# Both batches' scores first, then two parts of the network, at each level

## The chip, the cores and the metric

The kernel runs on 1 core of one Trainium2 chip. The metric is the device time of an execution in microseconds (us), the median of the runs. The core's engines work side by side, each through its own list of instructions in order: TensorE (PE; its weight loads are listed as PEld), VectorE (DVE), ScalarE (ACT), GpSimd (POOL) and SyncE (SP), which here only starts transfers. They wait for one another on semaphores.

## What is computed

A linear attention with a decaying state (4 batches, 8 heads, 768 steps, 48 channels a head), then two gated networks on the 3072 tokens of 384 channels. Everything is float32.

```python
for t in range(S):                     # the attention
    cur = einsum('bhd,bhe->bhde', u * kt, vt)
    y[:, :, t] = einsum('bhd,bhde->bhe', rt, state + cur)
    state = wt[..., None] * state + einsum('bhd,bhe->bhde', kt, vt)

xn = x / sqrt(mean(x * x) + 1e-6) * rms_g        # first network, width 1536
x  = (silu(xn @ w_gate) * (xn @ w_val)) @ w_out
h  = maximum(maximum(x @ w1, x @ w2), x @ w3)    # second network, width 768
out = h @ w_out2
```

## The kernel before

**Tiles and levels.** The 768 steps are cut into 6 tiles of 128. In a tile the attention of two batches at a time, a duo, is worked out in 7 levels by doubling: at level l the 128 steps are blocks of 2h = 2^(l+1), and the right half of each block sees its left half. `rB[j]` holds batch j's r (j is 0 or 1 in the duo; two rows of partitions hold the even and the odd heads), `kT[b]` its k, `wT[b]` the decays of the blocks. Per level and batch:

- TensorE's `scores` (L503) multiplies kT with the right halves of rB into the bank `ps_sc[:, j]`, eight matmuls for four pairs of heads; level 0 has none. It waits for both rescales of the level before and for the copy of the level before out of the same bank.
- VectorE's `rescale_r_even` (L913) and GpSimd's `rescale` (L1168 for k, L1175 for the odd heads' r) multiply by the block's decay. They wait for the level's scores and for the block decays of the level before.
- VectorE's `take_scores` (L938, at the last level L946) copies the scores that belong to the level into `A`, masked.
- VectorE's `double_blocks` (L925) makes the decays of the doubled blocks; it waits for all three rescales.

After the last level come the transposes of k (`k_token_major`, L540), the output (`attended`, L522 and L527), the update of the state (L549), and VectorE's terms for a token and its neighbour (`own_term`, `neighbour_term`; the latter behind levels 4 and 5). GpSimd multiplies r and k (`r_times_k`, L1146) behind level 5.

**The slots.** The first network for the tile before is spread over the attention. Its 36 parts come in threes for each of 12 columns f of the hidden layer: gate (f), value (f), output (f - 1), nine matmuls each (L484 to L486, each product split into three of high and low halves). A duo has 18 slots, two at each level (2l and 2l + 1) and four behind them, and each slot takes the next part. `part` exists on four engines: ScalarE makes the sigmoid of the gate (L703) and the high half of the hidden values (L707), VectorE the products with gate (L888, which frees the gate's bank) and value (L891), GpSimd the low half (L1139). All engines run the slots in the same order, and what stands in an engine's list ahead of a step holds it up. Tile 0 has no network yet in its first duo; there ScalarE and VectorE split weight pieces in some slots (`weights_early`; L876, L878). In tile 0's second duo each slot has two parts, on 256 tokens, and a weight piece with each odd part; tile 1's parts too have 256 tokens, those of later tiles 512. Slot 0 of tile 0's second duo also makes the transposed and split x (L741, L1040). The tiles 2 to 4 are one loop. After the last tile come the remaining pass of the first network and the second network.

**What sets the order.** The order is written out by hand in each engine's `duo_steps`. On TensorE and GpSimd a level is: batch 0's scores (or rescale), slot 2l, batch 1's, slot 2l + 1. On VectorE: rescale and copy of batch 0, slot 2l, rescale and copy of batch 1, doubling of batch 0, slot 2l + 1, doubling of batch 1.

Of the kernel before, what the change touches and what calls it, by code (L numbers as in the profile page):

```python
# [45 lines left out]
def rwkv_moe_kernel(nc, rc, kc, wc, r, k, v, u, g_w1, v_w1, o_w1, rms_g, w1, w2, w3, o_w2, out):  # L46
# [17 lines left out]
    with ExitStack() as ctx:  # L64
# [178 lines left out]
        def k_nth(a, duo, level, j):  # L243

            return step(duo, level, j) + 1 - (2 * duo if last_tile(a) else 0)
# [233 lines left out]
        def _(pe):  # L479
# [8 lines left out]
            def scores(a, duo, level, j):  # L488
                if level == 0:
                    return  # L490
                h = 1 << level
                after(pe, r_even_scaled, a, STEPS, r_nth(a, duo, level - 1, j))
                after(pe, r_odd_scaled, a, STEPS, r_nth(a, duo, level - 1, j))
                after(pe, k_scaled, a, STEPS, k_nth(a, duo, level - 1, j))
                if level == 1 and duo and last_tile(a):
                    after(pe, scores_used, a, SCORES, score(duo - 1, LEVELS - 1, j) + 1)
                elif level == 1:
                    after(pe, u_taken, a, B, 2 * duo + j - 1)
                else:
                    after(pe, scores_used, a, SCORES, score(duo, level, j) - 1)  # L500
                for q in range(PAIRS):
                    rights = rB[j][:, :, q, :].rearrange("p o (n two h) -> p o n two h", two=2, h=h)[:, :, :, 1, :]
                    last = mm(ps_sc[:, j, q * T:(q + 1) * T], kT[2 * duo + j][:, q, :], rights, start=True, stop=True)  # L503
                last.then_inc(scores_done, 1)
# [101 lines left out]
            def duo_steps(a, duo, slot):  # L606
                for level in range(LEVELS):
                    for j in range(2):
                        scores(a, duo, level, j)
                        slot(2 * level + j)  # L610
                k_token_major(a, duo, 0)
                k_token_major(a, duo, 1)
                attended(a, duo, 0)
                slot(TAIL_AT)
                state_update(a, duo, 0)
                attended(a, duo, 1)
                slot(TAIL_AT + 1)
                state_update(a, duo, 1)
                slot(TAIL_AT + 2)
                slot(TAIL_AT + 3)  # L620
# [57 lines left out]
        def _(act):  # L678
# [73 lines left out]
            def duo_steps(a, duo, slot):  # L752
                for level in range(LEVELS):
                    for j in range(2):
                        if level == LEVELS - 1:
                            copy_r_left(a, duo, j)
                        slot(2 * level + j)
                k_back(a, duo, 0)
                k_back(a, duo, 1)
                slot(TAIL_AT)  # L760
                squares(a, duo, 0)
                slot(TAIL_AT + 1)
                squares(a, duo, 1)
                slot(TAIL_AT + 2)
                slot(TAIL_AT + 3)
# [100 lines left out]
        def _(dve):  # L866
# [175 lines left out]

            def duo_steps(a, duo, slot):
                for level in range(LEVELS):
                    rescale_r_even(a, duo, level, 0)
                    take_scores(a, duo, level, 0)
                    slot(2 * level)
                    rescale_r_even(a, duo, level, 1)
                    take_scores(a, duo, level, 1)
                    double_blocks(a, duo, level, 0)  # L1050
                    slot(2 * level + 1)
                    double_blocks(a, duo, level, 1)
                    if level in NEIGHBOURS_AT:
                        neighbour_term(a, duo, NEIGHBOURS_AT.index(level))
                own_term(a, duo, 0)
                slot(TAIL_AT)
                add_y(a, duo, 0)
                decay_state(a, duo, 0)
                add_to_state(a, duo, 0)
                normalise(a, duo, 0)  # L1060
                own_term(a, duo, 1)
                slot(TAIL_AT + 1)
                add_y(a, duo, 1)
                decay_state(a, duo, 1)
                slot(TAIL_AT + 2)
                normalise(a, duo, 1)
                add_to_state(a, duo, 1)
                slot(TAIL_AT + 3)
# [62 lines left out]
        def _(pool):  # L1131
# [52 lines left out]
            def duo_steps(a, duo, slot):  # L1184
                for level in range(LEVELS):
                    for j in range(2):
                        rescale(a, duo, level, j)
                        slot(2 * level + j)
                    if level == LEVELS - 2:
                        r_times_k(a, duo, 0)  # L1190
                times_u(a, duo, 0)
                r_times_k(a, duo, 1)
                times_u(a, duo, 1)
                slot(TAIL_AT)
                inverse_rms(a, duo, 0)
                slot(TAIL_AT + 1)
                inverse_rms(a, duo, 1)
                slot(TAIL_AT + 2)
                slot(TAIL_AT + 3)
# [78 lines left out]
```

## Time and profile before

| | |
|---|---|
| median of 3 runs | 1040.18 us (1038.83 to 1042.09) |
| the profiled execution | 1042.37 us, span 1040.6 us, mean granted clock 0.985 |
| TensorE busy | 997.7 us (96%), 5680 matmuls |
| TensorE weight loads | 882.3 us (85%) |
| VectorE | 623.3 us (60%) |
| ScalarE | 246.2 us (24%) |
| GpSimd | 489.2 us (47%) |

Times in the rows are counted from the span's start. A busy share is an average over stages with different limits, so the stretches matter: the attention fills the first 650 us, in which VectorE and GpSimd have most of their work. A row of the timeline gives start, duration, engine, line, operation, output and inputs, shapes and count; in brackets the idle time before it and what ended it, where there was some.

### The profile page before, as it was taken

Reading aid. Unit: us, or ns where it says so; the run is one execution under the profiler, and the core shown is the slowest. Engines: PE = TensorE matmul, PEld = TensorE weight load, DVE = VectorE, ACT = ScalarE, POOL = GpSimd, SP = SyncE. Lnnn points to the kernel's source line nnn. Section 1 sums busy time; section 2 is a strip of 40 time slices with the busy share of each in tenths; the row PEclk is TensorE's granted clock in tenths of the full one; section 3 lists DMA queues with packets and bytes.
Section 4 is the critical chain, followed back from the end, with each engine's and each line's share of the span. In section 5 each row is a group of like instructions: output and inputs, shape, how many; then the busy total and the mean of one; then the engine's idle time right before and its main releaser. Section 6 shows DMA issues by size and latency. Waiting matters only on the chain.

```text
span 1040.6 us, 16737 instructions
## 1 busy us (share of the span) xinstructions
PE 997.7 (96%) x5680; PEld 882.3 (85%) x5680; DVE 623.3 (60%) x1047; ACT 246.2 (24%) x488; POOL 489.2 (47%) x540
## 2 busy tenths in 40 slices
PE   4778988899999999999999999999999999999998
PEld 4778988888888888888888888888888888888988
DVE  7878798988776877778776867444332212121221
ACT  2132312222123121222122212333322212121211
POOL 7656586857574757566674757212010201011111
PEclk9689999999999999999999999999999999999999
DMA  6533312212112120303021220201301010101000
GB/s 200 161 89 96 97 46 77 74 50 96 58 60 63 55 97 3 108 12 133 18 88 34 91 63 5 92 31 61 122 0 61 1 61 8 53 15 45 23 8 31
DMA packets 36221, 64.65 MB, mean 62 GB/s; under 512 B 4928, under 2 KB 22720, under 8 KB 36160
## 3 DMA queue, kind: packets, MB, share of 16 engines
q1 hardware_dynamic: 30288, 52.12, 15.2%
q10 hardware_dynamic: 5872, 11.80, 3.5%
q8 instruction: 28, 0.46, 0.2%
q14 instruction: 33, 0.27, 0.1%
HBM read 54.46 MB, written 9.44 MB: 61 GB/s over the span
## 4 chain that ended last, share of the span: by engine, by line
PE 84%; DVE 5%; POOL 5%; issue 3%; ACT 1%; DMA 0%; SPq 0%; ACTq 0%; POOLq 0%; DVEq 0%
PE ps_sc L503 10%; PE ps_acc L484 8%; PE ps_acc L486 8%; PE ps_acc L485 8%; PE ps_gate L484 6%; PE ps_gate L486 6%; PE ps_val L484 6%; PE ps_gate L485 6%; PE ps_val L486 5%; PE ps_val L485 5%; PE ps_desk L527 3%; PE ps_sc L486 2%; PE ps_sc L484 2%; PE ps_sc L485 2%; POOL kT L1168 2%
## 5 line engine op out<-in xcount | busy, mean ns | idle before, releaser
L503 PEld LDWEIGHTS ps_sc<-rB,kT 128*128 128x128 f32 x1152 | 155.8, 202 | 36.8 <-DVE rB L913 18.0
L503 PE MATMUL ps_sc<-rB,kT 128*128 128x128 f32 x1152 | 162.2, 288 | 25.8 <-DVE A L938 10.6
L1168 POOL TENSOR_TENSOR kT<-kT,wT 128x256 f32<-128x256 f32 x164 | 140.0, 853 | 83.9 <-PE ps_sc L503 56.4
L1236 POOL TENSOR_TENSOR h_lo<-h2f,h_hi 128x512 fp32r<-128x512 f32 x36 | 46.3, 1285 | 247.5 <-ACT h_hi L857 247.5
L1139 POOL TENSOR_TENSOR h_lo<-act_h,h_hi 128x512 fp32r<-128x512 f32 (+1 forms) x83 | 97.7, 1178 | 108.8 <-ACT h_hi L707 104.2
L1175 POOL TENSOR_TENSOR rB<-rB,wT 64x256 f32<-64x256 f32 x144 | 121.1, 841 | 11.3
L913 DVE TENSOR_TENSOR rB<-rB,wT 64x256 f32<-64x256 f32 x144 | 96.1, 672 | 30.4 <-PE ps_sc L503 23.7
L484 PE MATMUL ps_gate<-x_hi,wg_hi 128*128 128x512 f32 (+1 forms) x252 | 97.0, 385 | 8.9 <-DVE act_h L888 6.9
L707 ACT ACTIVATE h_hi<-act_h 128x512 fp32r<-128x512 f32 (+1 forms) x84 | 47.9, 571 | 230.4 <-DVE act_h L891 230.2
L938 DVE COPY_PREDICATED A<-mask,ps_sc 128x512 f32<-128x512 uint8 x120 | 98.9, 824 | 0.0
L484 PE MATMUL ps_acc<-h_hi,wo_hi 128*128 128x512 f32 (+1 forms) x252 | 95.7, 380 | 0.5 <-POOL h_lo L1139 0.3
L484 PE MATMUL ps_val<-x_hi,wv_hi 128*128 128x512 f32 (+1 forms) x252 | 96.2, 382 | 0.0
L703 ACT ACTIVATE act_h<-ps_gate 128x512 f32<-128x512 f32 (+1 forms) x84 | 45.1, 536 | 212.8 <-PE ps_gate L486 212.6
L486 PE MATMUL ps_gate<-x_hi,wg_lo 128*128 128x512 f32 (+1 forms) x252 | 91.8, 364 | 0.0
L486 PE MATMUL ps_val<-x_hi,wv_lo 128*128 128x512 f32 (+1 forms) x252 | 91.7, 364 | 0.0
L485 PE MATMUL ps_gate<-x_lo,wg_hi 128*128 128x512 f32 (+1 forms) x252 | 91.2, 362 | 0.0
L485 PE MATMUL ps_val<-x_lo,wv_hi 128*128 128x512 f32 (+1 forms) x252 | 91.1, 362 | 0.0
L925 DVE TENSOR_TENSOR wT<-wT 128x128 f32<-128x128 f32 (+6 forms) x160 | 77.1, 490 | 23.4 <-POOL rB L1175 21.5
L486 PE MATMUL ps_acc<-h_hi,wo_lo 128*128 128x512 f32 (+1 forms) x252 | 90.9, 361 | 0.0
L485 PE MATMUL ps_acc<-h_lo,wo_hi 128*128 128x512 f32 (+1 forms) x252 | 90.5, 359 | 0.0
L1115 DVE TENSOR_TENSOR h2f<-h2f,ps_val 128x512 f32<-128x512 f32 x18 | 12.4, 688 | 106.2 <-PE ps_val L486 106.2
L891 DVE TENSOR_TENSOR act_h<-act_h,ps_val 128x512 f32<-128x512 f32 (+1 forms) x84 | 51.4, 612 | 35.4 <-PE ps_val L486 34.1
(136 smaller groups left out, 2028.7 us busy)
## 6 DMA issues: line engine op xcount, KB each, us to landing
kT<-in_k_channels SPq DMA_DIRECT2D x24, 256.0 KB, 3.4
wT<-in_w_channels SPq DMA_DIRECT2D x24, 256.0 KB, 4.0
rB<-in_r_channels SPq DMA_DIRECT2D x48, 128.0 KB, 2.6
kL<-in_k_tokens SPq DMA_DIRECT2D x24, 192.0 KB, 2.4
rL<-in_r_tokens SPq DMA_DIRECT2D x24, 192.0 KB, 2.5
vL<-in_v_tokens SPq DMA_DIRECT2D x24, 192.0 KB, 2.4
x_scratch<-x1s SPq DMA_DIRECT2D x6, 768.0 KB, 4.4
xn<-x_scratch SPq DMA_DIRECT2D x6, 768.0 KB, 4.3
```

Of the source, the lines that this page charges most:

```text
L484: mm(dst, lhs[0], rhs[0], start=start, stop=False)
L485: mm(dst, lhs[0], rhs[1], start=False, stop=False)
L486: return mm(dst, lhs[1], rhs[0], start=False, stop=stop)
L503: last = mm(ps_sc[:, j, q * T:(q + 1) * T], kT[2 * duo + j][:, q, :], rights, start=True, stop=True)
L707: nc.scalar.activation(h_hi[:, f % 2, toks], act_h[:, f % 2, toks], ACT.Copy).then_inc(h_hi_done, 1)
L891: tt(hidden, hidden, ps_val[:, toks], ALU.mult).then_inc(val_used, 1)
L913: tt(new, old, block_decay(2 * duo + j, 1 << level, 0, HEAD_ROWS[0]), ALU.mult).then_inc(r_even_scaled, 1)
L925: tt(left, left, half(w[:, :, :], h, 1)[:, :, 0:1], ALU.mult).then_inc(tot_done, 1)
L938: nc.vector.copy_predicated(dst, every_head.broadcast_to([P, H, n, h]), src.rearrange("p (g n h) -> p g n h", g=H, h=h)).then_inc(scores_u ...
L1139: tt(h_lo[:, f % 2, toks], act_h[:, f % 2, toks], h_hi[:, f % 2, toks].bitcast(F32), ALU.subtract).then_inc(h_lo_done, 1)
L1168: tt(half(kT[b][:, :, :], h, 0), half(kT[b][:, :, :], h, 0), block_decay(b, h, 1), ALU.mult).then_inc(k_scaled, 1)
L1175: tt(new, old, block_decay(b, h, 0, HEAD_ROWS[1]), ALU.mult).then_inc(r_odd_scaled, 1)
```

## The change

In each engine's `duo_steps` the two batches' steps of a level come first and the level's two slots behind them. On VectorE the doublings of both batches also come ahead of both slots. On ScalarE the two copies of r (last level alone) come ahead of the last level's two slots. Instructions, waits and buffers are the same; only their order in the lists changes.

```diff
--- before
+++ after
@@ TensorE, duo_steps @@
                 for level in range(LEVELS):
                     for j in range(2):
                         scores(a, duo, level, j)
+                    for j in range(2):
                         slot(2 * level + j)
@@ ScalarE, duo_steps @@
                     for j in range(2):
                         if level == LEVELS - 1:
                             copy_r_left(a, duo, j)
+                    for j in range(2):
                         slot(2 * level + j)
@@ VectorE, duo_steps @@
                 for level in range(LEVELS):
-                    rescale_r_even(a, duo, level, 0)
-                    take_scores(a, duo, level, 0)
-                    slot(2 * level)
-                    rescale_r_even(a, duo, level, 1)
-                    take_scores(a, duo, level, 1)
-                    double_blocks(a, duo, level, 0)
-                    slot(2 * level + 1)
-                    double_blocks(a, duo, level, 1)
+                    for j in range(2):
+                        rescale_r_even(a, duo, level, j)
+                        take_scores(a, duo, level, j)
+                    for j in range(2):
+                        double_blocks(a, duo, level, j)
+                    for j in range(2):
+                        slot(2 * level + j)
@@ GpSimd, duo_steps @@
                     for j in range(2):
                         rescale(a, duo, level, j)
+                    for j in range(2):
                         slot(2 * level + j)
```

## Rows read from the trace of the kernel before

**Rows 1.** Windows: start:end, length, then busy us (instructions) of PE, PEld, DVE, ACT, POOL; clock.

```profile
83.00:86.50 3.50, 3.50 (x20) 3.50 (x19) 2.66 (x4) 2.02 (x3) 2.63 (x3) 0.54 0.43 123
...
174.00:222.70 48.70, 43.62 (x351) 41.87 (x352) 42.72 (x81) 11.92 (x30) 34.23 (x42) 1.00 0.21 66
336.20:449.70 113.50, 113.50 (x673) 99.42 (x673) 87.56 (x155) 26.48 (x54) 72.09 (x80) 1.00 0.19 63
```

**Rows 2.** Waits of TensorE: waiter, releaser, us in total, times, longest.

```profile
PE ps_sc L503 <- DVE A L938: 10.6, 7, 3.1
...
PE ps_gate L484 <- DVE act_h L888: 6.9, 5, 1.9
```

**Rows 3.** Timeline of TensorE in tile 3: start us, us, engine, line, op, tiles, count.

```profile
336.26 1.98 PE L503 MATMUL ps_sc<-rB,kT 128*128 128x128 f32 x16
337.99 0.48 PE L484 MATMUL ps_gate<-x_hi,wg_hi 128*128 128x512 f32 x1
...
340.17 1.05 PE L503 MATMUL ps_sc<-rB,kT 128*128 128x128 f32 x8
340.97 0.48 PE L484 MATMUL ps_val<-x_hi,wv_hi 128*128 128x512 f32 x1
...
369.81 1.03 PE L540 MATMUL ps_sc<-ident,kT 128*128 128x128 f32 x8
...
386.12 0.39 PE L484 MATMUL ps_gate<-x_hi,wg_hi 128*128 128x512 f32 x1
...
388.16 0.39 PE L484 MATMUL ps_val<-x_hi,wv_hi 128*128 128x512 f32 x1
```

**Rows 4.** Timeline of all engines in tile 3, first duo, levels 1 and 2.

```profile
340.93 1.31 DVE L938 COPY_PREDICATED A<-mask,ps_sc 128x512 f32<-128x512 uint8 x1
...
345.33 0.69 DVE L891 TENSOR_TENSOR act_h<-act_h,ps_val 128x512 f32<-128x512 f32 x1
...
346.06 0.63 ACT L707 ACTIVATE h_hi<-act_h 128x512 fp32r<-128x512 f32 x1 [5.10 <-DVE act_h L891]
...
346.76 1.29 POOL L1139 TENSOR_TENSOR h_lo<-act_h,h_hi 128x512 fp32r<-128x512 f32 x1 [0.36 <-ACT h_hi L707]
```

**Rows 5.** Timeline of VectorE in tile 1, second duo, levels 2 and 3.

```profile
182.58 0.42 DVE L891 TENSOR_TENSOR act_h<-act_h,ps_val 128x256 f32<-128x256 f32 x1
182.91 0.41 DVE L913 TENSOR_TENSOR rB<-rB,wT 64x256 f32<-64x256 f32 x1
...
184.82 0.86 DVE L925 TENSOR_TENSOR wT<-wT 128x64 f32<-128x64 f32 x1 [0.71 <-POOL rB L1175]
```

**Rows 6.** Timeline of GpSimd in tile 1, second duo, levels 0 to 5.

```profile
174.80 0.92 POOL L1175 TENSOR_TENSOR rB<-rB,wT 64x256 f32<-64x256 f32 x1
...
184.81 0.74 POOL L1139 TENSOR_TENSOR h_lo<-act_h,h_hi 128x256 fp32r<-128x256 f32 x1
...
187.11 0.85 POOL L1168 TENSOR_TENSOR kT<-kT,wT 128x256 f32<-128x256 f32 x1
...
188.78 0.65 POOL L1168 TENSOR_TENSOR kT<-kT,wT 128x256 f32<-128x256 f32 x1
...
198.94 1.49 POOL L1146 TENSOR_TENSOR prod<-rL,kL 128x384 f32<-128x384 f32 x1
```

**Rows 7.** Timeline of TensorE in tile 1, second duo: scores and transposes.

```profile
183.30 1.06 PE L503 MATMUL ps_sc<-rB,kT 128*128 128x128 f32 x8
...
191.25 1.06 PE L503 MATMUL ps_sc<-rB,kT 128*128 128x128 f32 x8
...
202.26 0.66 PE L540 MATMUL ps_sc<-ident,kT 128*128 128x128 f32 x4 [1.05 <-DVE A L946]
```

**Rows 8.** Timeline of GpSimd in tile 0, first duo: an odd rescale.

```profile
26.22 1.57 POOL L1175 TENSOR_TENSOR rB<-rB,wT 64x256 f32<-64x256 f32 x1
```

**Rows 9.** Timeline of all engines in tile 0, second duo, level 0.

```profile
57.71 0.55 PE L484 MATMUL ps_gate<-x_hi,wg_hi 128*128 128x256 f32 x1 [0.98 <-ACT x_hi L741]
...
63.20 0.95 DVE L913 TENSOR_TENSOR rB<-rB,wT 64x256 f32<-64x256 f32 x1
```

## The prediction

> **What bounds the kernel now.** I read the windows first. In tile 3, which stands for the tiles 2 to 5, TensorE is busy for 113.5 of 113.5 us and VectorE for 87.6 [rows 1]: TensorE is the bound, and the reader should see that the other engines have some 20% of slack, no more. In the second half of tile 1 (its network parts work on 256 tokens instead of 512) the picture turns: VectorE is busy for 42.7 of 48.7 us, close to TensorE's 43.6 [rows 1]. There and in tile 0 the bound changes from level to level. The list of TensorE's waits says on whom: 10.6 us in 7 places for the copies of the scores (L938), 6.9 us in 5 places for the gate product of VectorE (L888) that frees the gate's bank [rows 2]. So the thing to look at is not how much work there is, which the change leaves alone, but what stands in front of what in the queues of VectorE and GpSimd, and how much slack each has.
>
> **The order on TensorE itself, tiles 2 to 5.** From the scores at 340.17 to the transposes at 369.81 there are ten pairs of one batch's scores and one part: 29.64 / 10 = 2.964 us a pair, 5.93 us a level [rows 3]. One batch's scores alone take 0.80 us (340.17 to 340.97). In the new order a level is both scores, a part behind them, and a part behind a part. All three are in the trace, because in the first duo one slot is empty and level 0 has no scores: both scores take 337.99 - 336.26 = 1.73 us (not 2 x 0.80: the first part overlaps the tail of the scores before it only once), a part behind scores 340.17 - 337.99 = 2.18, a part behind a part 388.16 - 386.12 = 2.04 [rows 3]. Sum 5.95 against 5.93: +0.02 to +0.03 a level. Changed levels of such kind: 5 in a first duo (level 1 is already paired there), 6 in a second, 11 a tile, 44 in four tiles: **+1.2 us**. If the part behind a part keeps its gain and the paired scores cost nothing extra, it is -0.12 x 44 = -5.3; that is the lower end.
>
> **The waits that appear in tiles 2 to 5.** Scores (2,1), level 2 of batch 1, now start 0.80 us behind those of (2,0) instead of 2.96. They need the copy of scores (1,1) out of the same bank. In tile 3 that copy runs from 340.93 for 1.31 us [rows 4], at the end of two rescales and two copies that VectorE does in one go. In the new order the doubling of level 0 is out of their way and GpSimd's low part no longer meets them, so I take the copy to end at about 341.5, where (2,1) could start at 340.97: +0.5 us in a first duo. In a second duo the same place gives +0.3. Four tiles: 4 x 0.8 = **+3.2**, between 0 (the rescale of batch 1 may run alone, 0.41 us, instead of beside GpSimd, 0.95 [rows 5, 9], and that closes the gap) and 8 (the whole step of 1.3 in first and 0.7 in second duos). Elsewhere in the level the slack holds, narrowly. GpSimd needs 188.78 - 187.11 = 1.67 us for a batch's two rescales [rows 6], so both are done 0.9 + 3.34 = 4.2 us after the level begins, and scores (l+1,1) want them at 5.95 + 0.80 = 6.75. The low part of the hidden values, 1.29 us with 512 tokens [rows 4], stands between the levels when VectorE has made the value product, which is now queued behind the doubling of batch 1, which waits for GpSimd's last rescale: 4.2 + 0.3 + two products of 0.69 + ScalarE's 0.63 [rows 4] = 6.5, then 1.3, and GpSimd starts the next level's rescales at 7.8 instead of 6.8. Then their end is 7.8 + 3.34 = 11.1 and the scores (l+2,1) want them at 12.7. So one such level costs nothing, and it comes every third.
>
> **Tile 1.** Here a part is half as long, and the same chain has no slack. From scores (3,0) at 183.30 to (5,0) at 191.25 two levels take 7.95 us, 3.98 each, set by TensorE [rows 7]. I walk the second duo with the durations of the rows. Scores (1,1) wait for GpSimd's rescale of batch 1, which ends at 174.80 + 0.92 = 175.72 [rows 6]: they can't start earlier than today, and the part that stood ahead of them now stands behind, up to +1.1 us. VectorE's products of gate and value, 0.42 us each [rows 5], move behind the doubling. At (2,0) the copy of (1,0) is late by 0.7 and at (2,1) that of (1,1) by 0.3; scores (3,0) come at 184.6 instead of 183.3. In level 2 the doubling of batch 1 waits for GpSimd as it does now (0.71 us of idle time in front of it at 184.82 [rows 5]); but gate and value product, which now fill the place between the two copies (182.58 [rows 5]), come only after it, at 186.1 to 186.9. ScalarE's copy (0.42) and GpSimd's low part (0.74, 184.81 now [rows 6]) end at 188.2, and only then GpSimd takes level 3: scores (4,0) at 189.8 instead of 187.3, +2.5 us. Levels 3 and 4 run at TensorE's rate or 0.5 us above it. In level 5 the same order of waits returns, and behind it stands GpSimd's product of r and k (1.49 us [rows 6]): the low part at 202.0, the product to 204.1, level 6's rescales from 204.1; the transposes begin at 202.26 today [rows 7] and get the second k at 206.6, which puts what follows them 3.3 us later; and the output of the second batch waits 0.4 us more for VectorE: **+3.7 us** for this duo (1 to 5.5). The first duo walked in the same way gives less, since its level 1 is paired already: **+1.7** (0 to 3).
>
> **Tile 0.** In the first duo TensorE has no parts; the change only moves the split of a weight piece (L878) from between the two doublings to behind them. Now it meets GpSimd's rescale of batch 1, which takes 1.57 us [rows 8] instead of 0.92 [rows 6], in the chain that sets the level. Behind the doubling it meets the next level's first rescale, which has more room: about 0.35 us a level for three levels, **-1.0** (-2 to 0). In the second duo each slot has two parts and two weight pieces. The split of x stands in slot 0; today VectorE makes it ahead of batch 1's rescale (63.20 [rows 9]), after the change behind both rescales and both doublings, and the second doubling waits for GpSimd until 57.9. The first gate part then starts at 59.65 instead of 57.71 [rows 9]: +1.9. After that VectorE sets the pace, with the same work; walking it level by level I get its arrival at level 3 within 0.3 us of today's, at level 5 1.3 later, and the transposes at 113.2 instead of 110.9: **+2.3** (-3 to +6). TensorE waits for the gate product in blocks of 3 to 4 us in place of at most 1.9 [rows 2].
>
> **The sum.** -1.0 + 2.3 + 1.7 + 3.7 + 3.2 + 1.2 = +11.1 us. The profiled execution took 1042.4 us (span 1040.6), which is 2.2 above the median of 1040.2; from 1042.4 I get 1053.5, on the median 1051.3. No instruction is added, and ScalarE's and SyncE's programs change nowhere else: SyncE's loads wait for outputs and state updates, which stand behind the last level in both orders.
>
> **A rule weighed.** VectorE's even rescale takes 0.41 us alone and 0.95 beside GpSimd's [rows 5, 9], so 0.5 us is lost where the two meet. The Trainium skill (SBUF — State Buffer, Who interferes with whom) says that a VectorE instruction with two SBUF inputs and a GpSimd instruction that reads SBUF exclude each other for a whole instruction, while one with an SBUF and a PSUM input doesn't contend. By that rule the new order is worse than my walk: it takes the two PSUM products out of the time in which GpSimd rescales and leaves only contending ones there. The trace agrees in direction; in size the loss of 0.5 is less than a whole rescale of GpSimd.
>
> **The rivals.** (a) The order costs nothing measurable: TensorE catches up in tile 1 because the copies come earlier than I walk them, and tile 0's loss is offset by its first duo. -1 + 0 + 1 + 0 + 0 + 1 = +1: 1041. For it speaks VectorE's and GpSimd's slack in tile 3; against it the 0.71 us wait in front of the doubling, which exists today. (b) Faster: parts behind parts at 2.04 us, and the batch 1 scores are no longer held up. Its place is the 44 levels of tiles 2 to 5, its price -5.3, and with -1.0 and -2.0 in tile 0 and nothing lost in tile 1 it gives 1032. It decides if both scores take less than 1.65 us behind one another; the row says 1.73. (c) The clock. In 83.0 to 86.5 TensorE ran at 0.54 of its clock, the 1.2 GHz level for nearly all of it, right behind the wait of 1.9 us [rows 2], and the 3.5 us held what takes about 2 at 2.4 GHz [rows 1]. Waits of 3 to 4 us in tile 0 may bring this two or three times more, at 1.5 us each: 1055. (d) The slack that I found in tiles 2 to 5 is not there: GpSimd falls behind in every third level, as in tile 1, by 0.7 us, and both waits at level 2 last longer. 4 tiles x 2 duos x 2 levels x 0.7 = +11 more: 1062.
>
> **How the numbers follow.** The forecast has 0.50, (a) 0.15, (b) 0.08, (c) 0.15, (d) 0.12. The bounds of the terms reach from 1036 to 1067 if all went one way, which they won't; leaving out (b) and the far half of (d), the range is 1040 to 1061. A measurement of this kernel can tell 0.3%, 3.1 us, from no change. Slower by more: the forecast (its own range is 1044 to 1059), (c) and (d): 0.77. Same: (a), 0.15. Faster: (b), 0.08.
>
> **What would show it.** Right: in tile 3 the pair of scores at 1.73 us and small waits for L938 in front of (2,1), a tile of some 114.6 us; in tile 1 a duo of some 3 us more, with GpSimd's low part right in front of a level's rescales; in tile 0 the first gate part about 2 us later. Wrong: tile 3 unchanged or shorter, or tile 1's waits for L938 gone without others in their place; then VectorE's order mattered less than I think, or the time when GpSimd gets both scores mattered more.

## The result and the profile after

The changed kernel takes 1052.87 us (median; 1052.70 to 1054.77) beside 1041.13 us for the kernel before (1038.83 to 1042.53): a ratio of 1.0119, 95% interval [1.0103, 1.0135]. It is slower by 1.2%. The profiled execution took 1053.0 us, its span is 1051.3 us, 10.7 more than before's 1040.6.

The page of the changed kernel: busy us of each engine, the granted clock of TensorE in 40 slices, and the chain of work that ended last.

```profile
PE 999.4 (95%) x5680; PEld 883.0 (84%) x5680; DVE 635.3 (60%) x1047; ACT 245.9 (23%) x488; POOL 476.1 (45%) x540
...
PEclk9679999999999999999999999999999999999999
...
PE 78%; POOL 9%; issue 6%; DVE 5%; ACT 1%; DMA 0%; POOLq 0%; SPq 0%; DVEq 0%; ACTq 0%
```

The same chain in the kernel before:

```profile
PE 84%; DVE 5%; POOL 5%; issue 3%; ACT 1%; DMA 0%; SPq 0%; ACTq 0%; POOLq 0%; DVEq 0%
```

The same instructions ran, and TensorE is busy nearly as long as before (999.4 and 997.7 us). What has grown is the part of the chain that isn't TensorE: GpSimd's share from 5 to 9%, and the time in which an engine waited for nothing that the profile shows ("issue") from 3 to 6%. To see where, I cut both spans at TensorE's first transposes of x (L564), with which each tile ends. (The lines of VectorE, GpSimd and ScalarE stand one or two lower in the changed kernel: L938 is L940, L925 is L927, L1175 is L1176.)

| stretch, us | before | after | difference | predicted |
|---|---|---|---|---|
| tile 0, first duo | 55.18 | 54.90 | -0.3 | -1.0 |
| tile 0, second duo and tail | 70.64 | 71.28 | +0.6 | +2.3 |
| tile 1 | 89.31 | 94.50 | +5.2 | +5.4 |
| tiles 2 to 4, each | 113.50 | 115.13 | +1.63 | +1.1 |
| tile 5 and the second network | 485.01 | 485.20 | +0.2 | +1.1 |

Windows of the changed kernel (busy us and instructions of PE, PEld, DVE, ACT, POOL; then clock, DMA share, GB/s): the second duo and tail of tile 1, and a tile like tile 3. They answer to the second and third of [rows 1].

```profile
176.20:228.30 52.10, 44.86 (x351) 42.34 (x352) 44.16 (x82) 11.81 (x30) 33.41 (x42) 1.00 0.19 62
343.50:458.50 115.00, 114.11 (x673) 99.76 (x672) 91.39 (x155) 26.45 (x54) 70.53 (x80) 1.00 0.19 62
```

In tile 1 the same 351 matmuls now lie in 52.1 us instead of 48.7, and neither TensorE nor VectorE is full: the time went into waits. TensorE's waits in the changed kernel (us in total, times, longest):

```profile
PE ps_sc L503 <- DVE A L940: 12.2, 11, 4.9
...
PE ps_gate L484 <- DVE act_h L890: 6.6, 4, 3.7
PE ps_sc L503 <- POOL rB L1176: 6.0, 8, 2.1
PE ps_gate L484 <- issue: 3.0, 1, 3.0
...
PE ps_sc L540 <- POOL kT L1169: 1.9, 2, 0.9
...
PE ps_desk L522 <- DVE xn L996: 1.6, 5, 0.5
```

The odd rescale's line in the kernel before:

```profile
PE ps_sc L503 <- POOL rB L1175: 2.5, 3, 1.4
```

Beside [rows 2] the waits for the copies and the gate product have hardly grown in sum. Those for GpSimd's odd rescale went from 2.5 to 6.0 us. New are one of 3.0 us ahead of the first gate part in tile 0 (the profile has no releaser for it), two of 0.95 us of the transposes for GpSimd's k in tile 1, and small ones of the output product (L522) for VectorE at the end of the duos. All of TensorE's waits in this list together went from 39.9 to 48.3 us.

### The profile page after: what moved, and what is told of

It reads as the page before. It is cut to its first block, busy times and chain, and to the rows that moved or that the text cites. A ratio compares the mean times of both kernels' runs of the same rounds, so it can differ in the third digit from the quotient of the medians.

```text
span 1051.3 us, 16735 instructions
## 1 busy us (share of the span) xinstructions
PE 999.4 (95%) x5680; PEld 883.0 (84%) x5680; DVE 635.3 (60%) x1047; ACT 245.9 (23%) x488; POOL 476.1 (45%) x540
## 4 chain that ended last, share of the span: by engine, by line
PE 78%; POOL 9%; issue 6%; DVE 5%; ACT 1%; DMA 0%; POOLq 0%; SPq 0%; DVEq 0%; ACTq 0%
PE ps_sc L503 9%; PE ps_acc L484 7%; PE ps_acc L486 7%; PE ps_acc L485 7%; PE ps_val L484 5%; PE ps_val L486 5%; PE ps_gate L484 5%; PE ps_val L485 5%; PE ps_gate L486 5%; PE ps_gate L485 5%; POOL kT L1169 4%; POOL rB L1176 3%; PE ps_desk L527 3%; PE ps_sc L484 2%; PE ps_sc L486 2%
## 5 line engine op out<-in xcount | busy, mean ns | idle before, releaser
L503 PE MATMUL ps_sc<-rB,kT 128*128 128x128 f32 x1152 | 155.3, 288 | 28.8 <-DVE A L940 12.2
L503 PEld LDWEIGHTS ps_sc<-rB,kT 128*128 128x128 f32 x1152 | 148.6, 201 | 37.9 <-DVE rB L915 18.4
L1169 POOL TENSOR_TENSOR kT<-kT,wT 128x256 f32<-128x256 f32 x164 | 134.8, 822 | 68.2 <-PE ps_sc L503 52.3
L1176 POOL TENSOR_TENSOR rB<-rB,wT 64x256 f32<-64x256 f32 x144 | 113.6, 789 | 11.3
L927 DVE TENSOR_TENSOR wT<-wT 128x128 f32<-128x128 f32 (+6 forms) x160 | 82.2, 528 | 57.4 <-POOL rB L1176 48.8
L915 DVE TENSOR_TENSOR rB<-rB,wT 64x256 f32<-64x256 f32 x144 | 95.3, 668 | 9.9 <-issue 4.5
L940 DVE COPY_PREDICATED A<-mask,ps_sc 128x512 f32<-128x512 uint8 x120 | 98.9, 824 | 0.0
L1116 DVE TENSOR_TENSOR h2f<-h2f,ps_val 128x512 f32<-128x512 f32 x18 | 12.4, 687 | 106.3 <-PE ps_val L486 106.3
L890 DVE TENSOR_TENSOR act_h<-act_h,ps_gate 128x512 f32<-128x512 f32 (+1 forms) x84 | 50.8, 605 | 33.7 <-ACT act_h L704 33.4
```

Source lines behind the costliest of these rows:

```text
L890: tt(hidden, hidden, ps_gate[:, toks], ALU.mult).then_inc(gate_used, 1)
L915: tt(new, old, block_decay(2 * duo + j, 1 << level, 0, HEAD_ROWS[0]), ALU.mult).then_inc(r_even_scaled, 1)
L927: tt(left, left, half(w[:, :, :], h, 1)[:, :, 0:1], ALU.mult).then_inc(tot_done, 1)
L940: nc.vector.copy_predicated(dst, every_head.broadcast_to([P, H, n, h]), src.rearrange("p (g n h) -> p g n h", g=H, h=h)).then_inc(scores_u ...
L1169: tt(half(kT[b][:, :, :], h, 0), half(kT[b][:, :, :], h, 0), block_decay(b, h, 1), ALU.mult).then_inc(k_scaled, 1)
L1176: tt(new, old, block_decay(b, h, 0, HEAD_ROWS[1]), ALU.mult).then_inc(r_odd_scaled, 1)
```

## The experiments

Each kernel changes the order of work and nothing else. They ran in several groups, each with the kernel before beside them (its medians were 1041.13 to 1042.33 us), so the ratios compare better than the times; places inside a kernel are read from its one profiled execution. The theory after the comparison was: the time is lost in VectorE's order, because the doubling of batch 1, which waits for GpSimd's last rescale, now has both products of the network queued behind it. The rivals were TensorE's order itself, VectorE's rescales meeting GpSimd's (contention), and the granted clock of TensorE. The last column is the mean of tiles 2 to 4, between the transposes of x.

| kernel | time, us | ratio to before, 95% | a tile, us |
|---|---|---|---|
| changed kernel | 1052.87 | 1.0119 [1.0103, 1.0135] | 115.13 |
| e1_vector_old | 1041.05 | 0.9993 [0.9983, 1.0003] | 114.35 |
| e3_tensor_old | 1068.93 | 1.0251 [1.0233, 1.0268] | 117.21 |
| e5_doubling_last | 1051.07 | 1.0081 [1.0064, 1.0098] | 114.28 |
| e6_split_first | 1053.13 | 1.0106 [1.0089, 1.0123] | 115.13 |
| e7_tensor_only | 1049.71 | 1.0069 [1.0048, 1.0090] | 115.42 |
| e8_pool_only | 1040.38 | 0.9989 [0.9974, 1.0004] | 113.52 |
| e9_paired_early | 1038.67 | 0.9968 [0.9958, 0.9978] | 113.51 |
| e10_doubling_ahead | 1042.21 | 0.9997 [0.9986, 1.0008] | 114.18 |
| e11_last_level_old | 1049.90 | 1.0080 [1.0063, 1.0097] | 114.40 |
| e12_vector_old_early | 1043.91 | 1.0023 [1.0013, 1.0034] | 115.18 |

**VectorE's order undone.** From the changed kernel:

```diff
-                    for j in range(2):
-                        rescale_r_even(a, duo, level, j)
-                        take_scores(a, duo, level, j)
-                    for j in range(2):
-                        double_blocks(a, duo, level, j)
-                    for j in range(2):
-                        slot(2 * level + j)
+                    rescale_r_even(a, duo, level, 0)
+                    take_scores(a, duo, level, 0)
+                    slot(2 * level)
+                    rescale_r_even(a, duo, level, 1)
+                    take_scores(a, duo, level, 1)
+                    double_blocks(a, duo, level, 0)
+                    slot(2 * level + 1)
+                    double_blocks(a, duo, level, 1)
```

> The change on TensorE, ScalarE and GpSimd, but VectorE's order as it was before (batch 0, slot, batch 1, doubling, slot, doubling). My theory, that VectorE's products queued behind batch 1's doubling (which waits for GpSimd) make the loss of tile 1, expects tile 1's loss of 5.2 us (two duos, +1.9 and +3.3) to shrink to under 2, and the 2.0 us that tile 0's first gate part came later to vanish, since the split of x stands ahead of batch 1's rescale again: 1041 to 1046 us in all. The rival, that the loss comes from TensorE asking for both batches' scores at once, whatever VectorE's order, expects 1050 or more, with the waits of TensorE for L938-like copies in the same places.

Measured: 1041.05 us; the loss is gone. TensorE's order loses nothing on the whole as long as VectorE keeps its own and GpSimd follows. It isn't free everywhere, though: tiles 2 to 4 still take 0.85 us each more than before (114.25 to 114.52), while tile 0 ends 4.7 us earlier (121.13 against 125.82), in part by the clock, as the last run below shows. In the medians gains and losses leave no difference. (The second network, which no kernel here touches, took 1.6 us longer in this one profiled execution than in the others; why, the trace doesn't show.)

**TensorE's order undone**, the other three engines as in the changed kernel:

```diff
                         scores(a, duo, level, j)
-                    for j in range(2):
                         slot(2 * level + j)
```

> The change on VectorE, GpSimd and ScalarE, but TensorE in its old order (batch 0's scores, part, batch 1's scores, part). If VectorE's order makes the loss, it is here in full or more, because batch 1's scores now also come a part later (2.2 us with 512 tokens, 1.1 with 256) and the doubling and both products wait for them: 1053 to 1075 us, with TensorE waiting for the gate product in most levels of tile 1. If asking for both scores at once makes the loss, this kernel loses nothing: 1039 to 1044 us.

Measured: 1068.93 us, worse than both. VectorE waits in the middle of its level for the scores of batch 1, which TensorE makes one part later, and now has no product to do meanwhile: both stand behind that wait. A tile takes 3.7 us more than before, of which 1.4 lie in the tail of each duo (from the transposes of k on). This is read from the profiled execution, which took 1061.96 us; the other four took 1067.3 to 1069.2, and where their further 5 to 7 us lie isn't shown. VectorE's new order costs 12 us with TensorE's new order and 27 without it (against the run with GpSimd's new order alone, below): it is the part that hurts, and TensorE's is what makes it bearable.

**The doubling of batch 1 put last**, the rest as in the changed kernel:

```diff
-                    for j in range(2):
-                        double_blocks(a, duo, level, j)
+                    double_blocks(a, duo, level, 0)
                     for j in range(2):
                         slot(2 * level + j)
+                    double_blocks(a, duo, level, 1)
```

> The changed kernel with one step moved: VectorE doubles batch 1 behind both slots instead of ahead of them, so the products no longer wait for GpSimd's last rescale. My theory expects the third-level gap of tile 1 (scores (4,0) late behind a low part that GpSimd makes right ahead of its rescales) to close by 0.5 to 1 us each, four in tile 1: tile 1 1.5 to 3 us shorter than after the change, but where a slot's value product waits for TensorE the doubling now waits too, up to 0.6 us a level in tiles 2 to 5: 1049 to 1053 us. The rival (TensorE's order) expects no difference: 1052.9 within 0.5.

Measured: 1051.07 us. In tiles 2 to 4 it brings back as much as undoing VectorE's whole order: 114.28 us a tile; the wait of up to 0.6 us a level that I had expected there doesn't come. In tile 1 the second duo's stretch from transposes to transposes (L540) falls from 47.52 to 45.18, close to before's 44.20. But tile 0's second duo is 2.0 us longer than in the changed kernel, and tile 1's tail 2.5, both with the clock lower: from 55 to 80 us its mean is 0.65 against 0.77, and in the tail this kernel's windows (columns as above) show:

```profile
206.00:209.00 3.00, 1.53 (x12) 1.33 (x13) 2.96 (x7) 0.81 (x2) 2.69 (x5) 0.99 0.41 131
209.00:212.00 3.00, 3.00 (x17) 3.00 (x16) 2.71 (x4) 0.80 (x2) 2.92 (x4) 0.50 0.08 12
212.00:215.00 3.00, 3.00 (x15) 3.00 (x15) 1.57 (x4) 0.82 (x3) 0.98 (x1) 0.50 0.52 175
```

For 6 us TensorE ran at 1.2 GHz and made 32 matmuls; the changed kernel did nearly the same ahead of it (1.61 us busy in the 3 us from 206 on) and stayed at 1.00.

**The low half of x split where it was** (tile 0, second duo):

```diff
                         take_scores(a, duo, level, j)
+                        if first_tile(a) and duo == 1 and level == j == 0:
+                            x_split_lo(0)
...
-            run_tile_0(duo_steps, weights_early, x_split_lo, part_and_weights, end)
+            run_tile_0(duo_steps, weights_early, nothing, part_and_weights, end)
```

> The changed kernel with the low half of x for tile 0's second duo made right behind batch 0's first rescale, where it was before the change. My working of tile 0 expects the first gate part 1.9 to 2.0 us earlier (57.5 instead of 59.45) and, as VectorE sets the pace there and has the same work, the transposes of that duo 0.5 to 2 us earlier: 1051 to 1052.5 us. The rival, that the delay is absorbed by VectorE being the bound of that stretch, expects the transposes at the same time as after the change: 1052.9.

Measured: 1053.13 us, no difference in the time that the interval could tell. The trace shows the step. The first gate part of the changed kernel, and then of this one:

```profile
59.45 0.55 PE L484 MATMUL ps_gate<-x_hi,wg_hi 128*128 128x256 f32 x1 [3.00 <-issue]
```

```profile
57.64 0.55 PE L484 MATMUL ps_gate<-x_hi,wg_hi 128*128 128x256 f32 x1 [0.98 <-ACT x_hi L742]
```

From the transposes of x the part starts 4.55 us later in the changed kernel and 2.52 here (before: 2.53), and the duo is shorter by as much (54.32 against 56.35 us up to L540). The profiled span is 2.0 less, but the medians don't show it: the other three runs of this kernel took 1052.69 to 1054.01 us, as the changed kernel does. So the step is shown, and what it is worth in time isn't.

**TensorE's new order alone**, on the kernel before:

```diff
                         scores(a, duo, level, j)
+                    for j in range(2):
                         slot(2 * level + j)
```

> Before with the new order on TensorE alone (VectorE, GpSimd, ScalarE as before). The run with only VectorE's order undone kept a pitch of 114.26 us a tile in tiles 2 to 4, 0.78 over before, all of it one wait of 0.62 us at scores (2,1) of the first duo. If this wait comes from TensorE taking both scores together, it is here too: 114.2 to 114.3 a tile, 1042 us. If GpSimd's new order was what kept it small (its low part no longer stands between its two rescales), GpSimd is late here in every third level and the pitch is 115 or more: 1045 us.

Measured: 1049.71 us and 115.42 us a tile: the second case, and dearer than I put it. GpSimd's timeline in tile 3 of this kernel, and TensorE's scores (2,1):

```profile
341.61 1.28 POOL L1140 TENSOR_TENSOR h_lo<-act_h,h_hi 128x512 fp32r<-128x512 f32 x1 [0.17 <-POOL rB L1176]
342.84 1.02 POOL L1169 TENSOR_TENSOR kT<-kT,wT 128x256 f32<-128x256 f32 x1
343.94 0.83 POOL L1176 TENSOR_TENSOR rB<-rB,wT 64x256 f32<-64x256 f32 x1
```

```profile
345.11 1.15 PE L503 MATMUL ps_sc<-rB,kT 128*128 128x128 f32 x8 [1.72 <-POOL rB L1176]
```

The low part of the hidden values (1.28 us) stands between the two batches' rescales, and the second batch's scores wait 1.72 us. With GpSimd's new order it stands behind both, and the wait is 0.52 to 0.62. So GpSimd's part of the change (with ScalarE's, which the two runs don't separate from it) earns about 1.1 us a tile once TensorE's is there.

**GpSimd's new order alone**, on the kernel before:

```diff
                         rescale(a, duo, level, j)
+                    for j in range(2):
                         slot(2 * level + j)
```

> Before with the new order on GpSimd alone. The second batch's rescale on GpSimd now stands ahead of the low part of slot 2l and waits for scores that TensorE makes a whole part later. If GpSimd's slack in tiles 2 to 5 takes this, the time is 1041 to 1042 us and only tile 1 grows by 1 or 2 us. If the low part is late for the output product, each tile shows waits for h_lo (L1139) in front of TensorE's part of the output, some 1 us a tile: 1046 us.

Measured: 1040.38 us, a tile as before. In tiles 2 to 5 GpSimd's slack takes it. That tile 1 would grow by 1 or 2 us was wrong: it took 87.98 us, 1.3 less than before. TensorE's waits for the low part sum to 5.6 us in 3 places, all before tile 2, and are made up elsewhere.

**VectorE's old order, with only the doubling of batch 1 ahead of slot 2l + 1:**

```diff
                     double_blocks(a, duo, level, 0)
+                    double_blocks(a, duo, level, 1)
                     slot(2 * level + 1)
-                    double_blocks(a, duo, level, 1)
```

> TensorE, GpSimd and ScalarE in the new order; VectorE in the old one but for one step: the doubling of batch 1 stands ahead of the second slot's product instead of behind it. The theory that the products cost because they are queued behind a doubling that waits for GpSimd expects most of the loss back: tiles 2 to 4 at 115.1 us instead of 114.26, the transposes of a second duo followed 0.36 us later by what comes after, tile 1 some 2.5 us longer; 1046 to 1047 us. The rival, that the loss comes from the product of slot 2l leaving its place between the two batches (both rescales then meet GpSimd's), expects 1041 to 1042.

Measured: 1042.21 us, 114.18 us a tile. **The theory falls in this form.** I had expected most of the loss back from this one move. It costs 1.6 us in tile 1 of the profiled execution (90.58 us from transposes of x to the next, against 88.97 with VectorE's order undone) and nothing in tiles 2 to 5; the ratios, 0.9997 and 0.9993, don't tell the two kernels apart. Taken with the doubling put last, the two make a clear pattern: in tiles 2 to 4, moving only the products away from between the batches costs nothing, moving only the doubling ahead costs nothing, and both together cost 0.8. VectorE's time in the doublings (busy us, mean ns, then the idle time in front of them in us and what ended it), in the changed kernel, with this one move, and with VectorE's order undone:

```profile
L927 DVE TENSOR_TENSOR wT<-wT 128x128 f32<-128x128 f32 (+6 forms) x160 | 82.2, 528 | 57.4 <-POOL rB L1176 48.8 <-POOL rD L1176 6.7 <-issue 1.2
```

```profile
L927 DVE TENSOR_TENSOR wT<-wT 128x128 f32<-128x128 f32 (+6 forms) x160 | 84.2, 548 | 38.8 <-POOL rB L1177 31.1 <-POOL rD L1177 5.2 <-issue 1.2
```

```profile
L927 DVE TENSOR_TENSOR wT<-wT 128x128 f32<-128x128 f32 (+6 forms) x160 | 87.7, 564 | 19.8 <-POOL rB L1177 17.3 <-issue 1.2
```

The wait exists in all of them, longest in the changed kernel, and it doesn't order them by itself: with this one move it is twice that of the last kernel (38.8 against 19.8 us), and the kernels take the same time. My reading is that the work which VectorE still has behind it decides: one product, with the other already done, fits into the slack; two don't, and where a part is half as long (tile 1) even one doesn't quite. The next run shows where in tiles 2 to 4 this happens: in the last level alone.

**VectorE's old order in the last level alone**, the rest as in the changed kernel:

```diff
+                    last = level == LEVELS - 1
...
                     take_scores(a, duo, level, 0)
+                    if last:
+                        slot(2 * level)
...
                     double_blocks(a, duo, level, 0)
+                    if last:
+                        slot(2 * level + 1)
                     double_blocks(a, duo, level, 1)
+                    if not last:
+                        slot(2 * level)
+                        slot(2 * level + 1)
```

> The changed kernel with VectorE's old order in the last level of each duo alone (products after the first copy and between the doublings). If the loss at the end of each duo (transposes to the end of the tail 0.3 to 0.4 us longer in tiles 2 to 4, 1.4 us in the second duo of tile 1) comes from the two products that stand between the last doubling and the first own term, it goes: 115.1 to 114.4 us a tile, and some 2 us in tile 1; 1052.9 - 4 x 0.7 - 2 = 1048 us. The rest of the loss, at the levels of tile 1 and tile 0, stays. If the last level is not its cause: 1052.9.

Measured: 1049.90 us and 114.40 us a tile as expected; tile 1 came out 1.5 shorter instead of 2. This settles the tails: in tile 3 they last 20.39 and 16.31 us here, to the hundredth as in the kernel before, against 20.73 and 16.72 in the changed kernel, while the levels keep the changed kernel's times. So nearly all that VectorE's order costs in tiles 2 to 4 lies in the last level. The end of a duo in tile 3, VectorE in the changed kernel and then with its whole order undone:

```profile
378.82 0.99 DVE L927 TENSOR_TENSOR wT<-wT 128x4 f32<-128x4 f32 x1 [0.86 <-POOL rD L1176]
379.72 0.67 DVE L890 TENSOR_TENSOR act_h<-act_h,ps_gate 128x512 f32<-128x512 f32 x1
380.43 0.69 DVE L893 TENSOR_TENSOR act_h<-act_h,ps_val 128x512 f32<-128x512 f32 x1
381.04 0.54 DVE L983 TENSOR_REDUCE diag<-prod 128x8 f32<-128x384 f32 x1
```

```profile
366.01 0.67 DVE L890 TENSOR_TENSOR act_h<-act_h,ps_gate 128x512 f32<-128x512 f32 x1
366.76 0.69 DVE L893 TENSOR_TENSOR act_h<-act_h,ps_val 128x512 f32<-128x512 f32 x1
367.37 0.58 DVE L927 TENSOR_TENSOR wT<-wT 128x4 f32<-128x4 f32 x1
368.03 0.55 DVE L983 TENSOR_REDUCE diag<-prod 128x8 f32<-128x384 f32 x1
```

With the products first, they fill the time until GpSimd is done, the doubling doesn't wait, and the first own term (L983) comes 1.54 us behind TensorE's transposes (366.49). In the changed kernel the doubling waits 0.86 us, runs beside GpSimd, and has the products behind it: the own term comes 3.20 us behind the transposes (377.84), and with it the sum (L996) for which the next output product (L522) waits. Tile 5 of the changed kernel shows the same from the other side: there the last level has no doubling (`double_blocks` returns), and the tails are 17.68 and 14.02 us against 18.01 and 13.93 before, so not longer in sum.

**VectorE's new order from tile 2 on**, its old one in tiles 0 and 1:

```diff
+                    later = not isinstance(a, int) or a >= 2
```

(slots between the batches where `later` is false, behind the doublings where it is true.)

> TensorE, GpSimd and ScalarE in the new order everywhere; VectorE in the old order in tiles 0 and 1 and in the new one from tile 2 on. If the terms are the places where the traces show them, tiles 0 and 1 are those of the run with VectorE's order undone (1041.0 us) and tiles 2 to 4 have the pitch of the changed kernel, 115.1 instead of 114.26: 1041.0 + 4 x 0.85 = 1044.4 us; of the 11.8 us by which VectorE's order is slower, 3.4 lie in tiles 2 to 5 and 8.4 in tiles 0 and 1. If a late start in tile 1 is what makes the later tiles slow, their pitch here is 114.3 and the time 1041.

Measured: 1043.91 us, 115.18 us a tile, and tile 1 as with VectorE's order undone (88.90 us against 88.97). Tile 0 ends 1.7 us later than there (122.82 against 121.13), in two executions whose orders are the same up to that point. The terms lie where the traces put them: 2.9 us in tiles 2 to 5, the other 9.0 of VectorE's order in tiles 0 and 1.

**The gain kept, the loss left out.** VectorE's order as before; TensorE, GpSimd and ScalarE in the new order where `paired` holds, in the old one elsewhere:

```diff
+        def paired(a, duo):
+            return isinstance(a, int) and (a == 0 or (a == 1 and duo == 0))
...
                         scores(a, duo, level, j)
-                        slot(2 * level + j)
+                        if not paired(a, duo):
+                            slot(2 * level + j)
+                    if paired(a, duo):
+                        slot(2 * level)
+                        slot(2 * level + 1)
```

> VectorE's order as before everywhere; TensorE, GpSimd and ScalarE take the new order only in tile 0 and in the first duo of tile 1, and the old one from there on. In the run with only VectorE's order undone, tile 0 ended 4.7 us earlier than before (121.1 against 125.8) and the first duo of tile 1 was 0.6 shorter, while the rest lost 0.2 and 0.8 a tile. If the parts add up, this kernel keeps the gain without the loss: 1041.8 - 5 = 1037 us. If tile 0's gain was the clock of that one execution (its mean in the stretch from 80 to 110 us was 1.00 against 0.94), it needn't come back: 1041.

Measured: 1038.67 us, 0.9968 [0.9958, 0.9978]: faster than both kernels, by 0.3% of the kernel before, and less than the parts added up. Tile 0's second duo with its tail takes 68.18 us (before 70.64), the first duo of tile 1 0.6 less, the rest is as before. Some 1.6 to 1.8 us of this are the clock: from 80 to 110 us its mean was 0.94 in the kernel before (the fall of [rows 1]) and is 1.00 here. That fall stayed away in all five profiled executions in which TensorE had its new order there and VectorE its old one (one of them with the doubling of batch 1 ahead), and the ten timed runs hold the gain. That this order keeps the fall away is a reading of these five, not shown in the timed runs, whose clock is known only as a mean.

## Why the prediction was right, and where its terms were off

The forecast was 1051.3 us; the kernel took 1052.9, and the sum for the profiled execution was 1053.5 against 1053.0. The sign, the place and most of the mechanism held, but that the sum came out so near is luck: the terms for tile 0's second duo and for TensorE's own order were too high, and against them stands one that was missing, the tails of tiles 2 to 4.

**Tile 1, +5.4 predicted, +5.2 measured.** The walk holds almost place by place up to scores (4,0): +1.9 in the first duo (1.7 predicted) and +3.3 from there on (3.7). The rows of the changed kernel, second duo, levels 2 to 4:

```profile
187.90 0.28 DVE L927 TENSOR_TENSOR wT<-wT 128x64 f32<-128x64 f32 x1 [0.75 <-POOL rB L1176]
188.09 0.41 DVE L890 TENSOR_TENSOR act_h<-act_h,ps_gate 128x256 f32<-128x256 f32 x1
188.54 0.42 DVE L893 TENSOR_TENSOR act_h<-act_h,ps_val 128x256 f32<-128x256 f32 x1
```

```profile
189.55 0.74 POOL L1140 TENSOR_TENSOR h_lo<-act_h,h_hi 128x256 fp32r<-128x256 f32 x1 [1.74 <-ACT h_hi L708]
190.25 0.85 POOL L1169 TENSOR_TENSOR kT<-kT,wT 128x256 f32<-128x256 f32 x1
```

```profile
191.94 1.13 PE L503 MATMUL ps_sc<-rB,kT 128*128 128x128 f32 x8 [0.51 <-POOL rB L1176]
```

The doubling waits 0.75 us as it did (0.71 in [rows 5]), both products come behind it, and GpSimd's low part stands right ahead of its rescales instead of between them ([rows 6]). Scores (4,0) start 15.8 us behind scores (1,0) of the duo; the walk had 15.9 (189.8 - 173.89), and before it was 13.4. Behind that the walk was coarser: the second k reaches the transposes 2.6 us later than before, where it had 3.3 to 3.4, and from there to the transposes of x another 0.7 us is lost, where it had 0.4.

**Tile 0, second duo, +2.3 predicted, +0.6 measured.** Its first step was right: the gate part starts at 59.45 (predicted 59.65, before 57.71 [rows 9]), which is 2.0 us later counted from the transposes of x. The run with the split at its old place got these 2.0 us back in its profiled execution, though not in its median. What I put behind the step, +0.4 us, was -1.4. The clock, which I had made a rival, is hardly a part of that. The wait and the windows of the changed kernel:

```profile
72.16 0.38 PE L484 MATMUL ps_gate<-x_hi,wg_hi 128*128 128x256 f32 x1 [3.71 <-DVE act_h L890]
```

```profile
70.00:73.00 3.00, 0.84 (x7) 0.84 (x8) 2.53 (x6) 0.41 (x2) 0.00 (x0) 1.00 0.00 0
73.00:76.00 3.00, 3.00 (x18) 3.00 (x17) 1.77 (x4) 1.93 (x4) 0.74 (x1) 0.55 0.44 136
```

A wait of 3.7 us was followed by a fall to 1.2 GHz for most of 3 us, as rival (c) had it; but it came once, not two or three times more, and it took the place of the fall at 83 to 86.5 in the kernel before [rows 1], which is gone. From 73 to 79 us (0.55 and 0.88) it takes 1.7 us; the old one took (1 - 0.54) x 3.5 = 1.6. Rival (c) counted the falls that would come and not the one that would go. Of the -1.4 some 0.7 to 0.9 may be the gain of taking both scores together, an estimate from the last run above (2.5 us shorter there, 1.6 to 1.8 of it the clock); the rest stays open.

**Tile 0, first duo, -1.0 predicted, -0.3 measured**, and that before the change acts: the first scores start at 8.65 instead of 8.94. The odd rescales did get shorter as I had said: the three that took 1.56 or 1.57 us (one in [rows 8]) take 0.64 to 0.72, and one other, at 31.42, has grown to 1.38. But the duo did not follow: its second scores start 4.15 us behind the first, where it was 3.46 (TensorE waits for GpSimd 2.08 us instead of 1.38). In the profiled executions here this duo ended anywhere from 53.0 to 56.3 us, with no pattern by the order, so a term of 1 us could not be seen.

**Tiles 2 to 5, +4.4 predicted, 4.9 measured in tiles 2 to 4 and about 0.1 in tile 5.** Three terms were off, and nearly cancel. *TensorE's own order*, +1.2, is nothing: four levels of the first duo in tile 3 take 23.80 us, or 5.95 each; in the run with VectorE's order undone they take 5.90, and before 5.94. The sum of [rows 3] was good to 0.05 us a level, which times 44 is more than the term itself. *The wait at scores (2,1)* is there in first duos:

```profile
348.95 1.15 PE L503 MATMUL ps_sc<-rB,kT 128*128 128x128 f32 x8 [0.52 <-POOL rB L1176]
```

Its size is the 0.5 us of the sum, and the level grows by 0.77 us in all (6.66 against 5.89). But it ends with GpSimd's rescale (347.74 + 0.88 = 348.62), with the end of VectorE's copy 0.4 us ahead of that (346.86 + 1.34 = 348.20), while the prediction had the copy last. The one in the second duo, +0.3, isn't there (+0.05 in six levels). *The tails*, +0.34 and +0.41 us a tile, were not in the sum. I had the mechanism for tile 1 ("the output of the second batch waits 0.4 us more for VectorE") and left it out where VectorE has slack on the whole. The run with the last level put back shows that this is what they are. In tile 5, which the sum counted like the others and which grew by only 0.1 us, there is no doubling and no such tail. The mean slack of a tile (20%, [rows 1]) says nothing about a place where three engines hand over to each other.

**The rivals.** (a), no change, and (b), faster, both rested on TensorE; the levels at 5.90 us with VectorE's order undone would give at most 2 us over 44 levels. (d) would have shown levels some 0.7 us longer all over tiles 2 to 5; in tile 3, beside the one at scores (2,1), the longest are one of 6.09 us in the first duo and one of 6.21 in the second (5.99 before, and 6.21 with VectorE's order undone too). The bounds given there are not the sum of the terms' own bounds: those add up to -9.3 and +23.7 us, so 1031 to 1064 on the median, in place of 1036 to 1067.

**The rule weighed.** The rule weighed in the prediction, from the Trainium skill (SBUF — State Buffer, Who interferes with whom), would have made VectorE's instructions with two SBUF inputs dearer. That came about in part. The 144 even rescales stayed as they were (96.1 us busy before, 95.3 after), but the doublings (77.1 to 82.2), the last level's even rescales (12.4 to 16.3) and a product of the neighbour terms (16.9 to 21.2) grew. The state's decay fell (14.3 to 11.2), and the two products with a PSUM input stayed (101.9 and 102.1). VectorE is busy 12.0 us longer in all (623.3 to 635.3), GpSimd 13.1 less. Against the rule the prediction said that a loss of 0.5 us is less than a whole rescale of GpSimd. That comparison was wrong, since the GpSimd instruction had begun first. Of the 144 even rescales of the kernel before, 70 start while a GpSimd instruction has at least 0.15 us left, and 68 of these take 0.41 us plus that remainder less 0.12 to 0.14 (the other two take 0.41); in the changed kernel all 74 do. At 63.20 in [rows 9] the remainder is 0.68 us:

```profile
63.01 0.87 POOL L1139 TENSOR_TENSOR h_lo<-act_h,h_hi 128x256 fp32r<-128x256 f32 x1 [5.17 <-ACT h_hi L707]
```

The even rescale takes 0.95, which is 0.41 + 0.68 less 0.14. The products with gate and value, which read PSUM, take 0.66 to 0.69 us with 512 tokens whether GpSimd is at work or not. Both agree with the rule. So what a meeting costs VectorE depends on how far GpSimd's instruction has got. How much of the kernel's loss contention carries was not separated; in tiles 2 to 4 it isn't the rescales standing one behind another, since the kernel with the doubling last has them so and loses nothing there by it.

## What to carry to other kernels

When an instruction that waits for another engine is moved ahead of work that doesn't, its engine stands idle (here 57.4 us in front of the doublings instead of 19.8), and all that stands behind it comes later: go through what is queued behind it at the end of the loop too, where the next phase wants its result, and not only in the steady level. A reordering of several engines is several changes with different signs: here TensorE's half alone cost 7 us, GpSimd's alone nothing, both together nothing, VectorE's on top 12, and the version that beats both kernels leaves VectorE's out and uses the others only in the part where TensorE isn't the bound throughout. Slack is used up once: two moves that are each free may cost together.

## What the runs showed of the chip

The granted clock falls to its lower level (1.2 GHz) behind some gaps and not behind others that look alike. In the kernel before, the gaps of 1.66 and 1.72 us in front of gate parts at 68.84 and 74.94 us left it at 2.4 GHz, and behind the one of 1.91 us at 82.13 it fell. With the doubling last TensorE was busy 1.53 of 3 us ahead of the fall at 209, and in the changed kernel 1.61 of 3 at the same place, with no fall; that tail is 2.5 us longer with it. In tile 0 a fall is worth 1.6 to 1.7 us, and small shifts of order moved it, doubled it or took it away. For a term of 2 us in a stretch with such gaps, a single profiled execution is no proof.
